# Thirteen pairs ahead of the MLP, and the powers of two of queries and keys made on GpSimd

## The reference

```
# q, k, v: (4 batches, 8 heads, 768 positions, 64)
scores = q @ k.T / sqrt(64); keep position j for i if j < 4 (a sink) or 0 <= i - j < 128
a = softmax(scores over kept); x = a @ v              -> x: (3072 tokens, 512)
h = x @ w_in (512 x 2048); g = h - tanh(h); x = g @ w_out (2048 x 512)
e = argmax(x @ w_gate + modality_bias[modality_id])   # one of 8 experts per token
out = softmax weight of e * (max(x @ w1[e], 0) @ w2[e])
```

## Time and profile before

| what | value |
|---|---|
| median of 3 runs | 1062.03 us (1060.99 to 1062.84) |
| profiled execution, its own time | 1065.34 us |
| its span, first to last instruction | 1063.4 us |
| PE busy | 979.7 us, 92% of the span |
| DVE busy | 649.2 us, 61% |
| ACT busy | 533.0 us, 50% |
| POOL busy | 413.3 us, 39% |
| mean granted TensorE clock | 0.970 |

### The profile page before, as it was taken

How to read it: one execution, slowest core, us unless ns; L and a number is a source line. 1 busy time by engine, 2 the same in 40 slices (tenths; PEclk the granted TensorE clock), 3 DMA queues, 4 the chain that set the end, 5 groups by cost and what they waited for, 6 DMA issues and landing times.

```text
span 1063.4 us, 23350 instructions
## 1 busy us (share of the span) xinstructions
PE 979.7 (92%) x7808; PEld 591.2 (56%) x7808; DVE 649.2 (61%) x1824; ACT 533.0 (50%) x1329; POOL 413.3 (39%) x605
## 2 busy tenths in 40 slices
PE   3647999999999999999999999999899999899996
PEld 2423444554554555555455455555576777677773
DVE  7565877767768767777866765547574324733331
ACT  4454776655646764655665555446512224522221
POOL 4555887524325533434642432200132322232322
PEclk9666999999999999999999999999999999999998
DMA  9502001102100212101110100051115112111111
GB/s 349 183 18 79 19 18 36 49 19 81 64 19 19 48 37 79 49 19 36 19 48 19 36 31 1 2 188 31 24 29 208 50 50 45 40 41 49 50 50 38
DMA packets 24371, 60.26 MB, mean 57 GB/s; under 512 B 9504, under 2 KB 9760, under 8 KB 22752
## 3 DMA queue, kind: packets, MB, share of 16 engines
q1 hardware_dynamic: 15392, 45.77, 13.2%
q0 software_dynamic: 5728, 13.43, 4.1%
q10 hardware_dynamic: 3168, 0.02, 0.2%
HBM read 45.35 MB, written 14.12 MB: 56 GB/s over the span
## 4 chain that ended last, share of the span: by engine, by line
PE 70%; DVE 14%; issue 5%; ACT 4%; POOL 3%; DMA 2%; DVEq 1%; ACTq 0%; POOLq 0%; SPq 0%
PE h_ps L772 18%; PE acc L828 18%; PE pt_ps L1897 5%; PE h_ps L1948 5%; PE acc L1948 5%; PE s_ps L1897 5%; PE s_ps L579 3%; PE x_out L727 3%; PE pt_ps L646 2%; PE s_ps L879 2%; DVE g_raw L793 1%; ACT probs L602 1%; ACT g_hi L803 1%; PE s_ps L772 1%; DVE qk_top L402 1%
## 5 line engine op out<-in xcount | busy, mean ns | idle before, releaser
L828 PE MATMUL acc<-w_out_all,g_hi 128*128 128x512 f16 x768 | 228.4, 379 | 0.0
L772 PE MATMUL h_ps<-xt_hi,w_in_all 128*128 128x384 f16 x960 | 197.5, 329 | 5.4 <-DVE g_raw L793 3.5
L828 PE MATMUL acc<-w_out_all,g_lo 128*128 128x512 f16 x384 | 146.0, 380 | 2.7 <-DVE g_lo L813 2.7
L772 PEld LDWEIGHTS h_ps<-xt_hi,w_in_all 128*128 128x128 f16 x960 | 91.0, 100 | 65.2 <-issue 8.6
L784 ACT ACTIVATE g_raw<-h_ps,batch_scale 128x384 f32<-128x384 f32 x120 | 69.6, 580 | 101.8 <-PE h_ps L772 101.8
L102 POOL TENSOR_TENSOR tick<-tick 1x1 f32<-1x1 f32 x83 | 15.5, 187 | 264.8 <-ACT y L1964 117.1
L828 PEld LDWEIGHTS acc<-w_out_all,g_hi 128*128 128x128 f16 x768 | 75.2, 98 | 77.7
L813 DVE SCALAR_TENSOR_TENSOR g_lo<-g_raw,batch_scale,g_hi 128x384 f16<-128x384 f32 x128 | 88.4, 690 | 41.9 <-ACT g_hi L803 40.5
L803 ACT ACTIVATE g_hi<-g_raw,batch_scale 128x384 f16<-128x384 f32 x128 | 79.0, 617 | 60.7 <-DVE g_raw L793 59.0
L661 POOL TENSOR_SCALAR_AFFINE_SELECT pt<-merged 128x512 f16<-128x512 f16 x96 | 65.3, 680 | 91.6 <-DVE merged L655 89.8
L772 PE MATMUL h_ps<-xt_lo,w_in_all 128*128 128x384 f16 x480 | 99.0, 329 | 0.0
(11 more groups left out here) (314 smaller groups left out, 2203.3 us busy)
## 6 DMA issues: line engine op xcount, KB each, us to landing
qk_raw<-in_qk SPq DMA_DIRECT2D x31, 454.0 KB, 3.3
raw<-in_w SPq DMA_DIRECT2D x16, 512.0 KB, 7.8
v_raw<-in_v SPq DMA_DIRECT2D x4, 1536.0 KB, 7.0
x_tokens<-x SPq DMA_DIRECT2D x24, 256.0 KB, 2.5
w_in_all<-in_w_in SPq DMA_DIRECT2D x4, 1024.0 KB, 8.8
w_out_all<-in_w_out SPq DMA_DIRECT2D x4, 1024.0 KB, 11.0
x_tokens<-g_raw SPq DMA_DIRECT2D x1, 1024.0 KB, 6.4
vs_raw<-in_v SPq DMA_DIRECT2D x24, 4.0 KB
```

The lines of the kernel that those rows point to most:

```text
L772: mm = eng.matmul(h_of(m, f), w16[0][:, f, x * DM + k * P:x * DM + (k + 1) * P], r[:, par, k, :], start=(i == 0), stop=(i == 3 * KD - 1))
L828: mm = eng.matmul(acc[t][:, :], l[f % 2][:, t * P:(t + 1) * P], w16[1][:, f, x * DM:(x + 1) * DM], start=(f == 0 and i == 0), stop=(f == N ...
```

## The change

ALONE goes from 14 to 13, and slot 24 of window 0 now scores a pair, so that window 0 scores 14 and all later windows are as before. `weigh_values` and `split_x` of pair 11 move from the window's slots to the end of `alone`. The maxima go to a double buffer and raise their own semaphore `qk_topped`; from group 1 on `qk_scales` runs on GpSimd as five dependent instructions on two columns (group 0 stays on VectorE, now in five instructions as well). The items of the conversions move: keys' maximum, powers of two and multiplication from 6g - 7 to 6g - 9, halves from 6g - 5 and 6g - 3 to 6g - 7 and 6g - 6. In `prepare_alone` the scaling of the values comes earlier and their halves later. In `alone` ScalarE and VectorE do `transpose_sinks` in the second item of a turn instead of the first.

```diff
-ALONE = 14
+ALONE = 13
@@ qk_top_of
-                exponent_step(eng, eng.tensor_reduce(qk_top[:, i:i + 1], ...))
+                need(eng, q["qk_scaled"], g - 1)
+                eng.tensor_reduce(qk_top[:, g % 2, i:i + 1], ...).then_inc(q["qk_topped"], 1)
@@ qk_scales
-            if E == "dve":
+            if E == ("pool" if g else "dve"):
+                step = chain(eng, q["qk_step"], QK_STEPS * g)
+                eng.wait_ge(q["qk_topped"], 2 * (g + 1))
                 need(eng, q["qk_mult"], 2 * (g - 2))
                 s = qk_scale[:, g % 2, :]
-                for i in range(2):
-                    one_exp = qk_exp[:, i:i + 1]
-                    exponent_step(eng, eng.tensor_scalar(one_exp, qk_top[:, i:i + 1].bitcast(I32), 255 * EXP1, None,
-                                                         ALU.bitwise_and))
-                    exponent_step(eng, eng.tensor_scalar(one_exp, one_exp, float(LOWEST * EXP1), float(HIGHEST * EXP1),
-                                                         ALU.max, ALU.min))
-                exponent_step(eng, eng.tensor_scalar(qk_half[:], qk_exp[:, 1:2], qk_exp[:, 0:1], 0.5, ALU.subtract, ALU.mult))
-                exponent_step(eng, eng.tensor_scalar(qk_half[:], qk_half[:], float(127 * EXP1), None, ALU.add))
-                exponent_step(eng, eng.tensor_scalar(s[:, 0:1].bitcast(I32), qk_half[:], 255 * EXP1, None, ALU.bitwise_and))
+                step(eng.tensor_scalar(qk_exp[:], qk_top[:, g % 2, :].bitcast(I32), 1.0 / EXP1, float(LOWEST), ALU.mult, ALU.max))
+                step(eng.tensor_scalar(qk_exp[:], qk_exp[:], float(HIGHEST), 0.0, ALU.min, ALU.add))
+                step(eng.tensor_scalar(qk_half[:], qk_exp[:, 1:2], qk_exp[:, 0:1], 0.5, ALU.subtract, ALU.mult))
+                step(eng.tensor_scalar(s[:, 0:1].bitcast(I32), qk_half[:], 127.0, float(EXP1), ALU.add, ALU.mult))
                 eng.tensor_scalar(s[:, 1:2].bitcast(I32), s[:, 0:1].bitcast(I32), -1.0, ...).then_inc(q["qk_scaled"], 1)
@@ sink_halves (GpSimd, batch 0)
-                    eng.wait_ge(q["qk_mult"], 6)
+                    eng.wait_ge(q["conv_lo"], 8)
@@ conversions
-                early = {1: (None, 0, 1, 2), 2: (4, 5, 7, 8), 3: (8, 9, 11, 12), 4: (14, 15, 17, 18)}
-                q_top, k_top, q_split, k_split = early.get(g, (6 * g - 9, 6 * g - 7, 6 * g - 5, 6 * g - 3))
+                early = {1: (None, 0, 1, 2), 2: (4, 5, 6, 7), 3: (8, 9, 10, 11), 4: (13, 14, 15, 16), 5: (19, 20, 21, 22)}
+                q_top, k_top, q_split, k_split = early.get(g, (6 * g - 11, 6 * g - 9, 6 * g - 7, 6 * g - 6))
@@ prepare_alone
-            if i == (3 if E == "dve" else 5) and E in ("dve", "pe"):       # spread
+            if i == (3 if E == "dve" else 4) and E in ("dve", "pe"):
-            if i == 6:                                                     # v_scales, v_multiply
+            if i == (4 if E == "dve" else 5):
-            if i == 7:                                                     # v_split
+            if i == 8:
-            if i == 8:                                                     # sink_multiply
+            if i == 9:
-            if i == 9:                                                     # sink_halves
+            if i == 11:
-            if i in (4, 6, 7, 8):                                          # weight_gram of w_in
+            if i in (5, 6, 7, 8):
-            w_in_at = (13, 15, 17, 19, 21, 23, 25)
+            w_in_at = (13, 15, 17, 19, 21, 23, 24)
-            if i in (23, 26):                                              # weight_split of w_out
+            if i in (22, 24):
-            if i == 26:                                                    # late_constants, VectorE
+            if i == 24:
@@ alone
-            weighed = {5: (1,), 6: (2,), 7: (4, 5)}                        # and r - 2 for r > 7
+            weighed = {5: (1,), 7: (2,), 8: (4, 5)}                        # and r - 2 for r > 8
-                    if i == 2 * r:
-                        stage(transpose_sinks, E, eng, r - 1)
+                    if i == 2 * r + (E in ("act", "dve")):
+                        stage(transpose_sinks, E, eng, r - 1)
...
+            if E == "pe":
+                weigh_values(E, eng, PPC - 1)
+            split_x(E, eng, PPC - 1)
@@ plan_slots
-                    if k not in ((8, 16, 24) if w == 0 else (6, 14, 22, 30)):
+                    if k not in ((8, 16) if w == 0 else (6, 14, 22, 30)):
@@ window
-                        stage(weigh_values, E, eng, ago(4))
+                        if w or k:
+                            stage(weigh_values, E, eng, ago(4))
-                        stage(split_x, E, eng, ago(5))
+                        if w or k > 1:
+                            stage(split_x, E, eng, ago(5))
```

More of the change, by code:

```diff
@@ L166, in front @@
         table_fill = sb("table_fill", [P, NT, 2], I32)
-        qk_top = sb("qk_top", [P, 2], F32)
+        qk_top = sb("qk_top", [P, 2, 2], F32)
         qk_exp = sb("qk_exp", [P, 2], I32)
@@ L194, in front @@
         names = ("small_in first_k_in vs_zero v_zero qk_in0 qk_in1 v_in vs_in zero_st fill_st masked "
-                 "qk_scaled qk_mult conv_hi conv_lo sink_zero sink_copied "
+                 "qk_topped qk_step qk_scaled qk_mult conv_hi conv_lo sink_zero sink_copied "
                  "one_set w_gram top_in top_ps top_out scaled_v scaled_w v_mult v_hi_done v_lo_done vs_mult vs_hi_done vs_lo_done "
@@ L401, in qk_top_of @@
                     eng.wait_ge(q["first_k_in"], 16)
-                exponent_step(eng, eng.tensor_reduce(qk_top[:, i:i + 1], qk_raw[g % 2][:, qk_cuts(a)[i]], AX.X, ALU.max,
-                                                     apply_absolute_value=True))
+                need(eng, q["qk_scaled"], g - 1)
+                eng.tensor_reduce(qk_top[:, g % 2, i:i + 1], qk_raw[g % 2][:, qk_cuts(a)[i]], AX.X, ALU.max,
+                                  apply_absolute_value=True).then_inc(q["qk_topped"], 1)
@@ L422, in qk_scales @@
                                   ALU.mult, ALU.add).then_inc(q["qk_scaled"], 1)
+        QK_STEPS = 4
         def qk_multiply(E, eng, a, hp):
@@ L1193, in prepare_alone @@
                 v_split(E, eng, 0, (i - 1) // 2 - 6)
-            if i in (4, 6, 7, 8):
-                weight_gram(E, eng, 0, (4, 6, 7, 8).index(i))
+            if i in (5, 6, 7, 8):
+                weight_gram(E, eng, 0, i - 5)
             if i == 10:
@@ L1211, in prepare_alone @@
                 batch_scales(E, eng, 0)
-            if i in (23, 26):
-                weight_split(E, eng, 1, (23, 26).index(i))
-            if i == 26:
+            if i in (22, 24):
+                weight_split(E, eng, 1, (22, 24).index(i))
+            if i == 24:
                 if E == "dve":
@@ L1280, in alone @@
                         score_pair(E, eng, r + 1)
-                    for of in weighed.get(r, (r - 2,) if r > 7 else ()):
+                    for of in weighed.get(r, (r - 2,) if r > 8 else ()):
                         stage(weigh_values, E, eng, of)
```

2 lines of the change are left out of this document (removed).

## The result

The changed kernel takes 1058.51 us in the median of 20 runs (1057.1 to 1059.72), the kernel before 1062.37 beside it: a ratio of 0.9964 [0.9955, 0.9973], 3.9 us less. The forecast was 1055.3. The profiled execution took 1057.21 us with a span of 1055.6. PE is busy 969.2 us (92%), DVE 618.7 (59%, 30.5 less than before), ACT 531.2, POOL 453.4 (43%, 40.1 more).

The account below looks back on a forecast made before the run. PE was taken as the bound from the MLP's start at 88.4 us, the order of dependent work before it. -2.8 + 1.3 - 3.0 - 4.0 + 1.75 = -6.75 from 1062.03 gave 1055.3 us; 8-in-10 range 1048.5 to 1062.

Parts of the forecast that it names:

- the side given 0.76: Whole kernel: faster than before by over 0.2% (2.1 us), given a chance of 0.76.
- rival 1: Before the MLP: the first part gains nothing, MLP starts at 88.4, sum -3.95, 1058.1 us; chance 0.25.
- First part: Before the MLP, with 13 pairs: MLP begins at 85.6 instead of 88.4, 2.8 us earlier (bounds 84.4 to 87.4).
- The pair moved: Window 0: the added pair's PE work, scores, transposes and value products, costs 1.3 us (bounds 1.0 and 1.9).
- DVE's chain gone: PE's sink waits shrink without DVE's eight instructions: 3.0 us less in window 0, 4.0 in windows 1 to 6.
- GpSimd's chain: Window 0: one of five added chains falls before GpSimd's full stretch and PE waits 1.75 us (bounds 0 and 8.75).
- rival 3: GpSimd becomes the bound, by chains ahead of pairs 6, 8, 11 and five in window 0: up to 1067.1; chance 0.12.
- Windows 1 to 6: Sink waits of 5.5 us, and what hangs on DVE's order behind them, shrink: 4.0 us less.
- GpSimd: nothing: Windows 1 to 6: 21 added chains, 37 us, fall on GpSimd's idle share and cost nothing.
- k_lo: Windows 1 to 6: if GpSimd's idle cover were gone, a chain would delay k_lo, needed by scores three slots later.
- The chain, 1.75: One five-step chain on GpSimd: taken as 1.75 us, bounds 1.35 to 2.35.
- rival 4: Blocked port: chain steps and DVE instructions block each other, up to 0.27 us per chain on PE's path; 1062.3; chance 0.05.

Follow-up runs that it names:

- second execution: The changed kernel run again unaltered, for a second profile: median 1058.12 us, ratio 0.9967 to the kernel before.
- chain alone: Kernel before, fourteen pairs and all items kept, with only the five-step chain on GpSimd and the maxima's double buffer: 1047.32 us, ratio 0.9871.
- both orders: Changed kernel with chains of groups 3 to 5 behind the values' product and groups 6 to 31 on their old items: 1040.47 us, ratio 0.9807.
- doubled chain: Kernel with both orders plus four more dependent GpSimd steps, result overwritten, ahead of each chain from group 6 on: 1048.26 us, ratio 0.9871.

## Why the prediction was right, and where it wasn't

The time, 3.9 us less, lies inside the range and on the side given 0.76, and nearer to rival 1 (the first part gains nothing, -3.95) than to the forecast of -6.75. It is right in part by luck, as the third item shows. Term by term:

- **First part, forecast -2.8, measured -0.45** (87.21 and 88.21 against 88.42 and 87.91). This is the step that failed. The order of events was right: the exponentials came at 25.82, 43.90, 51.62, 62.98, 71.38 and 79.15 where 25.8, 44.0, 51.2, 62.3, 70.9 and 78.4 were forecast, and the steps to pairs 8 and 11 grew as said (7.72 and 8.40). Two sizes were off: the last exponential was 0.75 late, and the last step took 8.06, not 7.2, with 0.86 us of it the row sum of 1.03 us in place of 0.17. The forecast weighed the blocking of DVE only for the chain's steps; here it came from a big GpSimd instruction, as it had before the change (0.92 us at 79.59). The Trainium skill (SBUF — State Buffer, "Who interferes with whom") says beside the rule given in the prediction that `copy` and `tensor_scalar`, where their operands allow it, use both port pairs and then block or are blocked for a whole instruction; the rows of 1.03 us, a `tensor_scalar` and a copy, agree, and that half of the rule had been left out. The second execution came 1.0 later still: 0.6 of it stands at pair 6 (38.44 against 37.84), the rest at pair 10, and its cause was not looked for. That the chains stand in the path was seen; that putting them later is worth 7 us of this part (80.90) was not.
- **The pair moved, +1.3, with DVE's chain gone, -3.0, and GpSimd's chain, +1.75, in window 0: forecast +0.05, measured +1.2.** The sink waits fell by 2.6 (3.2 to 0.6); the prediction's 3.8 counted one wait twice, in the earlier trace rows and in the earlier trace rows. PE's waits on GpSimd's selects (0.5 before, 2.7 now) are the 1.75 and more. Over the runs the term comes apart otherwise than forecast: the chain alone takes 1.4 off window 0, thirteen pairs with the chains later take off another 1.3 though a pair is added (both orders), and the moved items of the windows cost 3.9. The doubled chain shows for the kernel with both orders that in window 0 all that is added on GpSimd is paid, not one chain in five: rival 3 had its place right. Its slower end did not come: it would decide from a chain of 1.72 us, the chain takes 1.61 in the median, and in windows 1 to 7 DVE without the chain gives back more.
- **Windows 1 to 6, -4.0: measured -4.5 (and +0.3 in window 7), by the wrong terms.** The sink waits fell by 3.2. But the chain's leaving DVE gave 9.5 (chain alone), and "GpSimd: nothing" was wrong by +5.2. The chain by itself is free there, nine tenths of it (doubled chain); what costs is what its new item put behind it, the values' product that ACT waits for. The forecast named k_lo as the one to be late; it was v_hi. Two errors of over 5 us, of opposite sign, met in one right number, which is luck.
- **The chain, 1.75: measured 1.62 to 1.63** in the first three; in the first part's other two 2.18 and 1.88, where a step took 0.80 instead of 0.24 and 0.58 instead of 0.32.
- **The blocked port (rival 4, 0.05)**: that the two engines hold each other up is seen, in the row sum and in the chain's step of 0.80, but a hold-up of 0.27 per chain on PE's path is not: four more such steps per group cost windows 1 to 7 2.2 us over 22 groups, 0.10 each.

The prediction took the 5.5 us of sink waits as nearly all that DVE's chain costs in windows 1 to 6, and bounded it by the 8.6 us of listed idle time. The chain alone gave 9.5: 6.9 of listed idle time and 2.6 of busy time. ACT's wait for DVE's gate in these windows fell as well, from 37.3 us before to 21.9 in the changed kernel and 23.4 with the chain alone. Which matmuls the 2.6 us stood in was not traced.

## What to carry to other kernels

Moving a chain of small dependent steps off an engine that feeds the bound one can be worth more than the bound one's idle time says (here 9.5 us against 8.6); do it alone first, with every other item where it was. A step that is moved along an in-order queue should be priced by what is queued behind it and who waits for that, even where its engine is idle more than half of the time. A change of several parts that comes out near nothing may hold one that is large: here the chain by itself gave 14 us, the whole change 4, and its parts in another order 21.

## What the hardware showed

- The full TensorE clock came 2.8 to 9.4 us after the start of the MLP, in executions of one program as in different ones; at 0.33 us per us (an estimate from two pairs of executions) that moves window 0 by up to 2.2 us, and has to be taken out before windows are compared.
- A VectorE instruction on 128 x 2 elements took 1.03 us instead of 0.17, and one on 128 x 72 1.03 instead of 0.20, beside a GpSimd operation with two inputs from SBUF, and ended with it. A step of GpSimd's chain was stretched alike, 0.80 for 0.24 at 48.05, beside a VectorE low half of w_in from 48.02 for 0.74.
- Five dependent steps on two and one int32 columns took 1.53 us on GpSimd from the first's start (10.51) to the last's end, and 0.99 on VectorE in the run with the chain back on DVE (from 10.44). The eight of the kernel before took 1.49 there.
